# Attention, a gated and a softplus feed-forward layer in fp32: loads in order of need, output weights loaded apart, x operands and second-stage weights earlier

## The reference

```python
kv = np.einsum('bhsd,bhse->bhde', k, v)
out = np.einsum('bhsd,bhde->bhse', q, kv)
x = out / np.sqrt(np.mean(out * out, axis=-1, keepdims=True) + 1e-06) * g_norm   # then heads side by side
g = x @ w_gate                                   # 512 -> 1536
x = (g / (1 + np.exp(-g)) * (x @ w_val)) @ w_out     # 1536 -> 512
h = x @ w_in2                                    # 512 -> 2048
out = (np.maximum(h, 0) + np.log1p(np.exp(-np.abs(h)))) @ w_out2
```

## Time and profile before

| | |
|---|---|
| median of 3 runs (lowest, highest) | 954.76 us (951.88, 955.02) |
| the profiled execution | 953.43 us |
| its span, first to last instruction | 951.6 us |
| TensorE busy | 897.7 us, 94% |
| VectorE, ScalarE, GpSimd busy | 678.0, 423.1, 241.4 us |
| mean granted clock of TensorE | 0.978 of 2.4 GHz |

### The profile page before, as it was taken

The page is one execution under the profiler, slowest core; times in us unless marked ns, Lnnn a source line. Parts: engine busy times, 40 slices in busy tenths (PEclk is TensorE's granted clock), DMA queues, the critical chain, the costliest instruction groups (busy, mean ns, idle before and its releaser), DMA issues.

```text
span 951.6 us, 14670 instructions
## 1 busy us (share of the span) xinstructions
PE 897.7 (94%) x5362; PEld 827.4 (87%) x5362; DVE 678.0 (71%) x1284; ACT 423.1 (44%) x742; POOL 241.4 (25%) x185
## 2 busy tenths in 40 slices
PE   8999798998899998899998799999999999999998
PEld 7999697998889898798987679899999999998997
DVE  3655444546796768887687489987887877878875
ACT  4527154463332333332232375454555545544643
POOL 4635003137950229950114432000000000000000
PEclk9999889898999999999998899999999999999999
DMA  9983636314210002210002330000000000000000
GB/s 266 215 232 91 144 92 148 99 38 119 78 34 1 1 13 67 67 46 1 2 1 93 110 108 1 1 33 0 33 0 0 33 0 0 33 0 0 34 1 34
DMA packets 95540, 53.92 MB, mean 57 GB/s; under 512 B 37248, under 2 KB 86528, under 8 KB 95488
## 3 DMA queue, kind: packets, MB, share of 16 engines
q1 hardware_dynamic: 95328, 53.23, 20.6%
q10 hardware_dynamic: 160, 0.00, 0.0%
HBM read 44.96 MB, written 8.26 MB: 56 GB/s over the span
## 4 chain that ended last, share of the span: by engine, by line
PE 74%; POOL 7%; DVE 7%; issue 4%; SPq 3%; DMA 3%; ACT 2%; DVEq 0%; POOLq 0%; ACTq 0%
PE bank L901 17%; PE bank L903 16%; PE bank L902 16%; PE bank L1060 7%; PE bank L1059 7%; PE bank L1058 7%; POOL slots L719 2%; SPq L506 1%; POOL slots L711 1%; PE bank L841 1%; POOL slots L715 1%; PE bank L834 1%; PE bank L909 1%; DMA v_rest<-in_v 1%; SPq L516 1%
## 5 line engine op out<-in xcount | busy, mean ns | idle before, releaser
L901 PE MATMUL bank<-x_hi,arena 128*128 128x384 f32 x554 | 189.6, 342 | 5.2 <-DVE act_a L1507 4.7
L903 PE MATMUL bank<-x_hi,arena 128*128 128x384 f32 x554 | 188.6, 341 | 0.0
L902 PE MATMUL bank<-x_lo,arena 128*128 128x384 f32 x554 | 187.9, 339 | 0.0
L901 PE MATMUL bank<-ring,slots 128*128 128x256 f32 x504 | 146.8, 291 | 25.9 <-ACT sum_a L1207 15.5
L903 PE MATMUL bank<-ring,slots 128*128 128x256 f32 x504 | 144.4, 287 | 0.0
L902 PE MATMUL bank<-ring,slots 128*128 128x256 f32 x504 | 144.4, 286 | 0.0
L1274 ACT ACTIVATE act_a<-bank 128x384 f32<-128x384 f32 x96 | 47.2, 492 | 177.1 <-PE bank L903 177.1
L901 PEld LDWEIGHTS bank<-ring,slots 128*128 128x128 f32 x504 | 98.2, 195 | 31.8 <-ACT sum_a L1207 17.1
L901 PEld LDWEIGHTS bank<-x_hi,arena 128*128 128x128 f32 x554 | 105.8, 191 | 10.7 <-DVE act_a L1507 5.1
L1058 PE MATMUL bank<-arena,g_hi 128*128 128x512 f32 x288 | 112.2, 390 | 2.3 <-DVE g_lo L1500 2.3
L1060 PE MATMUL bank<-arena,g_lo 128*128 128x512 f32 x288 | 113.1, 393 | 0.0
(11 more groups left out here) (138 smaller groups left out, 1663.6 us busy)
## 6 DMA issues: line engine op xcount, KB each, us to landing
stage<-in_moe_w_out SPq DMA_DIRECT2D x28, 256.0 KB, 3.3
out_dram<-out_stage SPq DMA_DIRECT2D x18, 256.0 KB, 2.1
k<-in_k SPq DMA_DIRECT2D x16, 256.0 KB, 3.3
v<-in_v SPq DMA_DIRECT2D x16, 256.0 KB, 3.1
stage<-in_moe_w_in SPq DMA_DIRECT2D x16, 256.0 KB, 2.8
xy<-in_q SPq DMA_DIRECT2D x48, 72.0 KB, 2.9
stage<-in_moe_w_gate SPq DMA_DIRECT2D x12, 256.0 KB, 3.7
stage<-in_moe_w_val SPq DMA_DIRECT2D x12, 256.0 KB, 3.9
```

Source lines behind the costliest of these rows:

```text
L901: nc.tensor.matmul(ps, hi, rhs_hi, start=first, stop=False)
L902: nc.tensor.matmul(ps, hi, rhs_lo, start=False, stop=False)
L903: return nc.tensor.matmul(ps, lo, rhs_hi, start=False, stop=last)
```

## The change

Nothing of TensorE's order changes. On the other engines:

- SP: the fetches of batch 1's tiles, the pairs 2 and 3 of batches 2 and 3, and the pairs 0 and 1 of batch 3 stand earlier, the q loads in their place later. `load7` is parted in `load7_up` and `load7_out`; the output weights of block f are issued after the gate and value weights of block f + 1, and those of block 1 so behind all stores and fetches of tiles.
- Output weights are made high in `weight_sum_highs`, one step later, and low last of all in `weight_lows`; a gate and value buffer is free after two low parts and the sums. Blocks 0 and 1 are made two steps earlier (`HIGH7_AT`).
- x operands: pieces 2 to 5 of a make stand in one run after `glu7` and before the split of the gated values; pieces 0 and 1 at steps 4, 9, 22, 27 (`EARLY_OF`; 4, 10, 22, 28 before). GpSimd starts the sums of a make three steps before the last of its predecessor. The ring is turned by one place, so that the slot of the second stage's block 13 is free after step 29.
- Second stage: the weights of ten blocks are made high in steps 31 to 35, two each, between `keep_p1` and the SiLUs (`HIGH2_AT`, `ORDER2`), their low parts by GpSimd; the high parts of the last six in the first chunk, their low parts by VectorE (`low_late`). The first x chunk is split one tile a step after steps 31 to 34.

```diff
-HIGH7_AT = {21: 0, 22: 1, 23: 2, 24: 3, 25: 4, 26: 5, 38: 6, 39: 7, 40: 8, 41: 9, 42: 10, 43: 11}
+HIGH7_AT = {19: 0, 20: 1, 22: 2, 23: 3, 25: 4, 26: 5, 38: 6, 39: 7, 40: 8, 42: 9, 43: 10, 44: 11}
+EARLY_OF = {4: 1, 9: 2, 22: 3, 27: 4}
+ORDER2 = (13, 0, 1, 2, 3, 4, 5, 6, 7, 8, 9, 10, 11, 12, 14, 15)
+LATE2 = 6
+SOON2 = NF2 - LATE2
+HIGH2_AT = {5 * SEG + 1 + n // 2: ORDER2[n:n + 2] for n in range(0, SOON2, 2)}
...
         load_q_blocks(2, 0)
         load_q_blocks(2, 1)
-        fetch_x(1, 2)
         keep_x(1, 3)
-        load_q_blocks(2, 2)
-        load_q_blocks(2, 3)
-        fetch_x(1, 3)
-        keep_x(1, 4)
         next_pair(2, 2)
         next_pair(2, 3)
+        fetch_x(1, 3)
+        load_q_blocks(2, 2)
+        keep_x(1, 4)
+        load_q_blocks(2, 3)
         fetch_x(1, 4)
...
-        load7(0)
+        sp.wait_ge(kv_done, B * KT)
+        load7_up(0)
+        load7_out(0)
         keep_x(3, 0)
         fetch_x(3, 0)
-        keep_x(3, 1)
-        fetch_x(3, 1)
-        load7(1)
-        for j in range(2, NT):
+        load7_up(1)
+        for j in range(1, NT):
             keep_x(3, j)
             fetch_x(3, j)
         for f in range(2, NF1):
-            load7(f)
+            load7_up(f)
+            load7_out(f - 1)
+        load7_out(NF1 - 1)
...
+            if m:
+                pool.wait_ge(p_done, product_count(LAST_STEP_OF_MAKE[m - 1] - 3, SEVEN - 1))
...
+        def weight_sum_highs(f):
+
+            act.wait_ge(s_sum_ready, 4 * (f + 1))
+            nc.scalar.activation(w7_part(f, 0, 3, SEVEN), w7_sum(f, 3, SEVEN), ACT.Copy).then_inc(w7_hi_ready, 1)
             act.wait_ge(raw7_out_loaded, 16 * (f + 1))
             nc.scalar.activation(slots7[:, f % SEG, OUT7:RAW7], raw7_out[:, :], ACT.Copy).then_inc(w7_hi_ready, 1)
...
             keep_p1(q)
+            for f in HIGH2_AT.get(q, ()):
+                split_high2(f)
             silu7(q)
...
-            for f in range(EARLY2):
-                if STEPS7 - SEG + under(f) + 1 == q:
-                    split_high2(f)
...
             glu7(q)
-            if q + 1 in TURN_OF:
+            if q in TURN_OF:
+                for i in range(2, 6):
+                    x7_low(TURN_OF[q], i)
+            split_g7(q)
+            if q in EARLY_OF:
                 for i in range(2):
-                    x7_low(TURN_OF[q + 1], i)
+                    x7_low(EARLY_OF[q], i)
...
+            if 0 < q - 5 * SEG <= KT:
+                split_x(NC1, bass.ds(0, CB), val_done, PLAIN, scaled=False, to=(x2_hi, x2_lo), tiles=[q - 5 * SEG - 1])
...
+        for f in range(NF2 - 1):
+            softplus(0, f)
+            if f % 2 and f // 2 < LATE2:
+                low_late(f // 2)
```

More of the change, by code:

```diff
@@ L87 @@
 LOWS7 = 5
+LOWS7_RAW = 2
 MAKE_OF = (0, 1, 2, 2, 3, 4)
@@ L364, in high_count2, with wait_low2 @@
     def high_count2(f):
-        return high_count(NF1 - 1) + f + 1
+        return high_count(NF1 - 1) + ORDER2.index(f) + 1
     def low_count2(f):
-        return low_count(NF1 - 1) + f + 1
+        return low_count(NF1 - 1) + ORDER2.index(f) + 1
+    def wait_low2(engine, f):
+        if ORDER2.index(f) < SOON2:
+            engine.wait_ge(w_ready, low_count2(f))
+        else:
+            engine.wait_ge(w_late_ready, ORDER2.index(f) - SOON2 + 1)
     def w2_in(f, part, i):
@@ L458, in raw_count2 @@
     def raw_count2(f):
-        return 32 * (f // 2 + 1)
+        return 32 * (ORDER2.index(f) // 2 + 1)
     def under(f):
@@ L468, in wait_slot2 @@
             engine.wait_ge(down_done, STEPS1 - SEG + under(f) + 1)
+        elif f == EARLY2:
+            engine.wait_ge(p_done, product_count(STEPS7 - SEG - 1, SEVEN - 1))
         else:
@@ L554, in load_step2 @@
         def load_step2(f):
-            if f < 2:
+            n = ORDER2.index(f)
+            if n < 2:
                 sp.wait_ge(w7_ready, LOWS7 * NF1)
             else:
-                sp.wait_ge(w_ready, low_count2(f - 2))
-            s = f % 2
+                wait_low2(sp, ORDER2[n - 2])
+            s = n % 2
             sp.dma_start(stage2[:, s, 0:KT * P].rearrange("p (t n) -> p t n", t=KT),
@@ L592, in _ @@
         keep_x(1, 0)
+        fetch_x(1, 0)
         load_step1(NF1 - 1)
-        fetch_x(1, 0)
         keep_x(1, 1)
@@ L637, in _ @@
         for f in range(2, NF1):
-            load7(f)
-        for f in range(NF2):
+            load7_up(f)
+            load7_out(f - 1)
+        load7_out(NF1 - 1)
+        for f in ORDER2:
             load_step2(f)
@@ L720, in weight_lows @@
                                         w7_part(f, 0, i, i + 2).bitcast(F32), ALU.subtract).then_inc(w7_ready, 1)
+            pool.wait_ge(w7_hi_ready, 3 * f + 3)
+            nc.gpsimd.tensor_tensor(slots7[:, f % SEG, RAW7 + OUT7:SLOT7], raw7_out[:, :],
+                                    slots7[:, f % SEG, OUT7:RAW7].bitcast(F32), ALU.subtract).then_inc(w7_ready, 1)
         def wait_x7_place(m, i):
@@ L756, in _ @@
         x_sums(4)
-        for f in range(NF2):
+        for f in ORDER2[:SOON2]:
             wait_slot2(pool, f)
-            low(high_count2(f), arena[:, slots2[f]:slots2[f] + SLOT2], stage2[:, f % 2, :], RAW2)
+            low(high_count2(f), arena[:, slots2[f]:slots2[f] + SLOT2], stage2[:, ORDER2.index(f) % 2, :], RAW2)
     @block.tensor
@@ L1038, in up2 @@
         def up2(c, f):
[L1040 removed]
+            wait_low2(pe, f)
             for t in range(KT):
@@ L1355, in _ @@
         softplus_terms(0, 1)
-        late2 = [f for f in range(NF2) if f >= EARLY2 or STEPS7 - SEG + under(f) + 1 == STEPS7]
         for f in range(2, NF2):
-            if f % 2 == 0 and late2:
-                split_high2(late2.pop(0))
+            if f % 2 == 0 and f // 2 <= LATE2:
+                split_high2(ORDER2[SOON2 + f // 2 - 1])
             softplus_terms(0, f)
-        assert not late2
         softplus_terms(1, 0)
@@ L1460, in normalize, with split_x @@
                                     ALU.mult).then_inc(xn_ready, 1)
-        def split_x(n, chunk, used, count, scaled=True, to=(x_hi, x_lo)):
-            for t in range(KT):
+        def split_x(n, chunk, used, count, scaled=True, to=(x_hi, x_lo), tiles=range(KT)):
+            for t in tiles:
                 if t < KT - 1:
@@ L1531, in glu7 @@
             a, b, c, d = [bank[BANK_OF[p]][:, early] for p in (P1, P6, P7, P5)]
-            turn, turned = TURN_OF.get(q), TURN_OF.get(q - 1)
+            turned = TURN_OF.get(q - 1)
             dve.wait_ge(p1_kept, q + 1)
@@ L1645, in _, with low_late, next_x @@
         dve.wait_ge(y_added, 2 * (KT - 1))
-        with dve.Fori(0, NCH - 1) as c:
+        def low_late(n):
+            f = ORDER2[SOON2 + n]
+            slot = arena[:, slots2[f]:slots2[f] + SLOT2]
+            dve.wait_ge(w_hi_ready, high_count2(f))
+            nc.vector.tensor_tensor(slot[:, RAW2:SLOT2], stage2[:, (SOON2 + n) % 2, :], slot[:, 0:RAW2].bitcast(F32),
+                                    ALU.subtract).then_inc(w_late_ready, 1)
+        def next_x(c):
+            split_x(c + (NC1 + 1), bass.ds(c * CB + CB, CB), hid_done, c * NF2 + NF2, scaled=False, to=(x2_hi, x2_lo))
+        for f in range(NF2 - 1):
+            softplus(0, f)
+            if f % 2 and f // 2 < LATE2:
+                low_late(f // 2)
+        next_x(0)
+        softplus(0, NF2 - 1)
+        with dve.Fori(0, NCH - 2) as c:
             for f in range(NF2 - 1):
-                softplus(c, f)
-            split_x(c + (NC1 + 1), bass.ds(c * CB + CB, CB), hid_done, c * NF2 + NF2, scaled=False, to=(x2_hi, x2_lo))
-            softplus(c, NF2 - 1)
+                softplus(c + 1, f)
+            next_x(c + 1)
+            softplus(c + 1, NF2 - 1)
         for f in range(NF2):
```

58 lines of the change are left out of this document (22 added, 36 removed).

## The result

| | before | after |
|---|---|---|
| median (lowest, highest) | 953.6 us (951.88, 955.02), 4 runs | 928.2 us (923.29, 929.55), 4 runs |
| the profiled execution | 953.43 us | 928.44 us |
| its span | 951.6 us | 926.4 us |
| mean granted clock | 0.978 | 0.982 |
| first seven-product step starts | 224.30 | 208.10 |

The ratio is 0.9725 (95% interval 0.9684 to 0.9766), so the change gains 25 us. The forecast was 917 us in a range of 899 to 933: the time is inside it, and 11 us above the forecast. It is also 2 us above the part of the range, 909 to 926, that the forecast's own mechanism was given. The two profiled spans differ by 25.2 us where the prediction's sum had 37.6.

What follows compares the result with a forecast made beforehand. TensorE's waits and the low clock after them were taken as the bound. Terms 8.8 + 7.3 + 0 + 11.6 + 8.3 - 1.6 + 3.2 = 37.6 off 953.43 gave 915.8, stated as 917 us; range 899 to 933.

Steps and rivals of the forecast that it cites:

- rival 2: Steps 32 to 35: collisions come twice a step and the clock falls, 17 us more, 926 to 936; chance 0.20.
- rival 3: Steps 14 to 23: GpSimd at 9.6 us a block sets the pace, x operands late too, 924 to 930; chance 0.10.
- Pairs of batches 2 and 3: Plain steps: late pairs loaded ahead of q loads; 8.8 us gained in batch 2, 7.3 in batch 3.
- the wait before the seven-product steps: Old wait for a late store goes (6.7), a new SiLU wait of 4 to 5.5 plus low clock comes; net 0.
- Output weights copied a step later: Steps 1, 2 and 17 to 20: ScalarE's waits go, 5.5 and 7.1 gained less 1.0 lost; 11.6 us.
- x operands earlier: Steps at each change of chunk (5, 6, 12, 24, 30): 8.3 us gained, step 5 keeping its 1.2.
- Second stage's weights and x: Steps 31 to 35: stalls of 15.7 removed, new waits and low clock of 17.3; net 1.6 lost.
- Rival 1: New waits do not bite: block 1's load lands early, VectorE's products get in first; 893 to 909; chance 0.17.
- Second stage (3.2): Second stage: six low parts move from GpSimd to VectorE, so the collisions there go; 3.2 us gained.
- Rival 4: Slower: TensorE's clock stays at its lower level from step 31 on, 955 to 960; chance 0.03.

Runs made afterwards that it cites:

- experiment 7: Kernel before with only SP's new load order from batch 1's first tile fetch to batch 2's fourth tile store (late pairs ahead of q loads): 935.71 us.
- experiment 1: Changed kernel with block 1 of the seven-product weights made high at step 21 instead of 20: 921.91 us.
- experiment 6: Changed kernel with GpSimd's third to sixth sums of x in makes 1 and 3 waiting for VectorE's low parts of pieces 0 and 1: 919.29 us.
- experiment 2: Changed kernel with the load of block 1's output weights issued ahead of the last tile's store: 919.16 us.
- experiment 3: Changed kernel with both second-stage weight copies of a step moved behind that step's SiLUs: 914.71 us.
- experiment 4: Changed kernel with only the second of a step's second-stage weight copies moved behind the SiLUs, the first left ahead: 907.74 us.
- experiment 5: Changed kernel with GpSimd's low parts of ten second-stage blocks replaced by a memset, leaving out those low parts: 912.33 us.
- experiment 8: Changed kernel with three edits: block 1's output load earlier, second copy behind the SiLUs, GpSimd's later x sums behind VectorE's first low parts: 895.68 us.

## Why the prediction was right in the main, and where it failed

**What was right and what the range held.** The waits, engines and orders that the prediction named came in all its items but two places, the x operands of step 5 and what GpSimd leaves for step 23; 25.2 of its 37.6 us were gained. That the time is inside the range is owed to its width: 928.2 lies above the forecast's own part (909 to 926) and in those of rival 2 (926 to 936) and rival 3 (924 to 930), neither of which came as described.

**Pairs of batches 2 and 3 (8.8 + 7.3) and the wait before the seven-product steps (0)**: together 16.2 us by the starts of the seven-product steps, 16.1 in the sum. Apart they were each a little off: the pairs alone gave 17.5 (experiment 7), so the third item was 1.3 lost, not 0, just outside its bound of 1 lost. Its mechanism came as worked out, load, copy, table load and SiLU in this order, with a wait of 5.7 for "4 to 5.5" and some 3.2 of low clock (experiment 1) for 2.0.

**Output weights copied a step later (11.6)**: steps 1 and 2 at 15.55, 5.5 gained, steps 17 to 20 at 31.12, 7.1 gained, as forecast. Rival 3 (GpSimd paces these steps) fell: GpSimd is busy for 29.27 of 31.12 us and holds nobody up. But where the sum took off 1.0, "I keep 1.0 of the 7.1 as lost there or in the x operands behind it", the loss behind was 7.3: GpSimd comes out of block 11 just in step 22, and its sums of x fall on VectorE's products, split and pieces 0 and 1, one after another (step 23).

**x operands earlier (8.3)**: steps 6 and 24 are at 7.78, as forecast; steps 12 and 30 gained 0.8 and 0.9 for 1.2 each. The step that failed is "The first two operands of make 1 stay where they were, with the 1.2 of step 5". They stand in the same place of the order, and step 5 lost 5.6 instead of 1.2 (2.9 in the four executions without low clock). The 1.2 was read as the price of a place in the order, while the rows of both kernels show the price of who started first (no run moved that start by itself): 0.6 us of shift turned one wait for an operation of GpSimd into two, and in this execution the clock fell after the longer wait of TensorE. Taking this one meeting away returned step 5 to 7.78 (experiment 6). The prediction weighed the port rule where the change adds low parts and did not apply it to the sums of x, which the change also moves. These two places, 4.4 and 6.3 us, are 10.7 of the 12.4 missing, and 2.8 of the 4.4 are low clock that most executions did not have.

**Second stage's weights and x (15.7 - 17.3)**: steps 32 to 35 with the last down product take 52.47. The sum had 3 x 7.78 and 10.6 for the undisturbed ones and 17.3 new, 51.2. The waits were 1.94 for "2.0" and 0.93 for "1.2" in each of the four steps. The chain ran 0.2 to 0.3 us behind the one worked out, and so did TensorE: the product ended at T + 4.1 for 3.9, its twin at 4.4 for 4.2, and P1 was kept at T + 4.92 for 4.65 (the copy starts at 4.54), while P2 could have started at T + 3.04 for 2.7. The low clock came as forecast in two steps: 32 and 34 take 12.7 at a granted clock of 0.87, step 33 with the same waits 11.16 at 1.00. Rival 1 (the waits do not bite) and rival 2 (two collisions a step) both fell. VectorE did win the race for the x split that rival 2 counted on:

```profile
475.97 0.56 DVE L1502 TENSOR_TENSOR x_lo<-xy,x_hi 128x384 fp32r<-128x384 f32 x1
...
476.04 2.74 POOL L696 TENSOR_TENSOR arena<-stage,arena 128x1024 fp32r<-128x1024 f32 x1 [2.19 <-ACT arena L1197]
```

by 0.07 us. The Trainium skill, SBUF - State Buffer, section "SBUF: two separate sides", says that the one of VectorE and GpSimd that starts first holds the shared port for its whole instruction; both orders of the race are in this trace, and both agree with it (0.28 us from GpSimd's end to VectorE's; here GpSimd's operation is the longer one, 2.74 for 2.42). The "about 927 without the clock" of rival 2 assumed that GpSimd wins each time: it wins one of the two races in each step here, and the 928.4 of the profiled execution is near that figure for another reason, steps 5 and 23.

**Second stage (3.2)**: 403.02 became 399.84, 3.2 gained. The six low parts on VectorE take 1.22 us each (estimated at 1.5 at most) and cost nothing, as forecast.

**Rival 4** (slower, the clock stays low): the clock came back every time, and the granted clock over steps 32 to 35 was 0.93.

Two readings are bounded only. The low clock behind step 23's wait varies: with the same wait of 4.8 the step takes 14.4 to 14.7 in experiments 1 to 5 and 15.06 here, so some 0.5 of its 7.3 is chance of the execution. And that GpSimd must come out of block 11 earlier to spare step 23 was not tried by itself.

## What to carry to other kernels

An operation that "stays where it was" is not priced by what it cost before, if the engine beside it moves: look for what shares its port in the new order, and ask who starts first, since a few tenths of a microsecond decide about a whole instruction. Give an engine's low-priority work the slots in which its partner works from PSUM, as experiment 4 did by moving one copy behind two short SiLUs for 20 us. Place a load by when it is needed, not behind a group that it belongs to: one DMA moved ahead of a tile's stores, its fetch and two loads of weights was worth 9 us (experiment 2).

## What the runs showed of the hardware

**A held operation does its work behind the holder.** An operation of VectorE that waits for one of GpSimd ends behind it by its own length less 0.15 to 0.19 us. Those that take 0.42 to 0.43 alone ended 0.27 to 0.28 us after GpSimd's (the product of step 32, the CAST of step 23), those that take 0.69 to 0.74 alone 0.54 to 0.55 (`g_lo` of step 23, 394.63 + 1.66 against 394.28 + 1.47; the last x operand ahead of the sum of step 5, 250.53 + 1.75 against 250.47 + 1.26). So a meeting costs what GpSimd's operation has left, less those 0.15 to 0.19.

**The memset did not hold VectorE up** (0.43 us beside it, against 2.44 beside a subtraction of the same width, experiment 5), and what it lacks is an operand to read from SBUF; no other such operation was tried. The Trainium skill, SBUF - State Buffer, section "SBUF: two separate sides", says the same: an operation of VectorE with two SBUF inputs is held up only by one of GpSimd that reads SBUF. I had read it as a rule on all of GpSimd's work. Of VectorE's, those with a PSUM operand kept their 0.41 to 0.42 in the rows above, while products of two SBUF operands, a CAST from SBUF to SBUF (1.40 for 0.43) and SCALAR_TENSOR_TENSOR (1.75 for 0.74) waited.

**The same wait does not always cost the same clock.** Step 5 has a wait of 2.58 to 2.60 us in the kernel after (above), in experiment 4 and in experiment 2:

```profile
246.11:258.25 12.14, 9.56 (x55) 8.75 (x54) 10.98 (x19) 5.00 (x9) 5.89 (x4) 0.86 0.01 1
```

```profile
237.14:247.77 10.63, 8.03 (x56) 7.34 (x55) 10.46 (x18) 4.50 (x9) 5.92 (x4) 1.00 0.00 0
```

The granted clock is 0.75, 0.86 and 1.00, that is some 6.7 us, 3.4 us and nothing at the 1.2 GHz level, and the step takes 13.42, 12.14 and 10.63. Experiments 1, 3 and 5 are like experiment 2 (10.61 to 10.66 at 1.00). What decides between the three was not found. It is a reason to read stretches at both levels before an edit is credited with a saving (experiment 8).
